# Two feed-forward networks over five token tiles in place of six, unrolled, with one buffer for the activated chunk

## The reference, cut to what matters

```python
def _attn_ref(q, k, v):                      # q, k, v: (4, 8, 1152, 64)
    q_pool = q.reshape(B, H, S // 2, 2, D).mean(axis=3)
    scores = scale * np.matmul(q_pool, k.transpose(0, 1, 3, 2))
    ...
    return np.matmul(attn, v)                # softmax over the keys

def _moe_ref(x, w_in, w_out):                # x: (2304, 512), w_in: (512, 2048)
    h = x @ w_in
    g = h * (1.0 / (1.0 + np.exp(-h)))
    return g @ w_out

def _moe2_ref(x, w1, w2, w3, w_out):         # w1, w2: (512, 1024), w3: (1024, 1024)
    a = x @ w1
    b = x @ w2
    h = a * b @ w3
    return h @ w_out                         # (2304, 512)
```

## Time and profile before

| | us |
|---|---|
| median of 3 runs | 1469.06 (1468.89 to 1470.64) |
| profiled execution: span from first to last instruction | 1465.5 |
| median less that span | 3.5 |
| TensorE busy | 1352.9 (92%) |
| VectorE busy | 799.6 (55%) |
| ScalarE busy | 697.3 (48%) |
| GpSimd busy | 434.8 (30%) |

### The profile page before, as it was taken

The page is one execution under the profiler, slowest core; times in us unless marked ns, Lnnn a source line. Parts: engine busy times, 40 slices in busy tenths (PEclk is TensorE's granted clock), DMA queues, the critical chain, the costliest instruction groups (busy, mean ns, idle before and its releaser), DMA issues.

```text
span 1465.5 us, 24978 instructions
## 1 busy us (share of the span) xinstructions
PE 1352.9 (92%) x8224; PEld 1296.8 (88%) x8224; DVE 799.6 (55%) x1340; ACT 697.3 (48%) x1266; POOL 434.8 (30%) x322
## 2 busy tenths in 40 slices
PE   6888888888888888889999999999999999999998
PEld 5887877787778787778899999999999899999998
DVE  7888888888888889888531111111114522122221
ACT  4776666666666666667742222222224422121211
POOL 4766656666655766655200000000000000000000
PEclk9999999999999999999999999999999999999999
DMA  6233323333323233320220000000104200000000
GB/s 155 73 81 81 95 64 80 81 79 81 91 68 81 68 92 81 79 72 24 61 65 8 1 1 1 1 0 0 43 0 153 92 1 22 23 22 1 21 21 22
DMA packets 33694, 76.34 MB, mean 52 GB/s; under 512 B 8944, under 2 KB 12144, under 8 KB 33648
## 3 DMA queue, kind: packets, MB, share of 16 engines
q1 hardware_dynamic: 33648, 75.73, 19.1%
HBM read 70.84 MB, written 4.79 MB: 52 GB/s over the span
## 4 chain that ended last, share of the span: by engine, by line
PE 77%; DVE 13%; issue 7%; DVEq 1%; DMA 1%; ACT 0%; SPq 0%; ACTq 0%
PE psum L907 21%; PE psum L908 20%; PE psum L909 20%; PE psum L923 5%; PE psum L924 4%; DVE mx L708 4%; PE psum L948 3%; PE psum L949 3%; DVE mneg L717 2%; DVE pL L726 2%; DVE mneg L719 2%; PE psum L932 1%; DVE kB L691 1%; DVE xT L732 1%; DVE qHs L702 1%
## 5 line engine op out<-in xcount | busy, mean ns | idle before, releaser
L708 DVE TENSOR_REDUCE mx<-psum 128x1 f32<-128x384 f32 (+1 forms) x480 | 253.1, 548 | 74.3 <-PE psum L924 73.7
L516 ACT ACTIVATE pF<-psum 128x576 f32<-128x576 f32 x288 | 187.7, 652 | 158.9 <-PE psum L949 156.8
L923 PE MATMUL psum<-kA,qHm 128*128 128x384 f32 (+1 forms) x480 | 172.4, 359 | 60.5 <-DVE mx L708 50.4
L836 DVE TENSOR_TENSOR gL<-gF,gH 128x384 fp32r<-128x384 f32 x96 | 53.6, 558 | 306.0 <-ACT gH L593 306.0
L424 POOL TENSOR_TENSOR pL<-pF,pH 128x576 fp32r<-128x576 f32 x93 | 143.0, 1538 | 216.8 <-ACT pH L522 216.7
L522 ACT CAST pH<-pF 128x576 fp32r<-128x576 f32 x288 | 194.5, 675 | 4.6
L726 DVE TENSOR_TENSOR pL<-pF,pH 128x576 fp32r<-128x576 f32 x195 | 187.6, 962 | 15.0 <-ACT pH L522 14.5
L907 PE MATMUL psum<-pH,vH 128*128 128x288 f32 x576 | 178.7, 310 | 1.5 <-DVE xT L732 0.7
L590 ACT ACTIVATE gF<-psum 128x384 f32<-128x384 f32 x96 | 47.3, 492 | 261.9 <-PE psum L909 261.9
L909 PE MATMUL psum<-pH,vL 128*128 128x288 f32 x576 | 171.0, 297 | 0.0
L908 PE MATMUL psum<-pL,vH 128*128 128x288 f32 x576 | 170.8, 297 | 0.0
(11 more groups left out here) (88 smaller groups left out, 3030.0 us busy)
## 6 DMA issues: line engine op xcount, KB each, us to landing
qraw<-in_qT SPq DMA_DIRECT2D x64, 288.0 KB, 4.2
kraw<-in_kT SPq DMA_DIRECT2D x64, 288.0 KB, 5.1
vraw<-in_v SPq DMA_DIRECT2D x32, 288.0 KB, 2.7
rsums<-recips SPq DMA_DIRECT2D x32, 144.0 KB, 2.9
outT<-oS SPq DMA_DIRECT2D x6, 768.0 KB, 3.4
wstage<-in_w_in SPq DMA_DIRECT2D x16, 256.0 KB, 3.4
fstage<-in_w3T SPq DMA_DIRECT2D x8, 512.0 KB, 4.7
w12stage<-in_w SPq DMA_DIRECT2D x8, 512.0 KB, 4.7
```

Of the source, the lines that this page charges most:

```text
L516: act.activation(two(pF[r][:]), stbank[(NC * j + c) % 2], ACT.Exp, scale=SCALE).then_inc(exp_done, 1)
L708: dve.tensor_reduce(mx[0:m, qt, b:b + 1], max_bank(h, jj, t)[0:m, 0:KW], AX.X, ALU.max)\
L923: pe.matmul(out, qHm[jj][:, cols], kA[jj][:, kblock(b)], start=True, stop=False)
```

## The change

The 2304 tokens are cut into five tiles: four of 464 columns and a last one of 448. All tile loops of both networks are written out, on all engines. `gF` has one buffer in place of two, so the silu of a chunk waits for the `gL` of the chunk before it. The order of the two `xH`, `xL` buffers is changed (the first network now begins with buffer 1), and `sums`, `rsums` and `ident` move into the memory of the attention stage; two waits are added for what now lies over them. The attention stage's instructions are the same.

```diff
-    TILE = 384
-    TILES = TOK // TILE
+    TILES = -(-TOK // 512)
+    TILE = -(-TOK // TILES // 16) * 16
...
-        ident = sb("ident", [P])
         wstage = sb("wstage", [WSLICE])
-        sums = sb("sums", [Q])
-        rsums = sb("rsums", [Q])
...
+            sums = sb("sums", [Q], F32, st)
+            rsums = sb("rsums", [Q], F32, st)
...
-        for j in range(2):
+        for j in (1, 0):
             xH[j] = sb(f"xH{j}", [KC, TILE], F32R, ffn)
             xL[j] = sb(f"xL{j}", [KC, TILE], F32R, ffn)
+            if j == 1:
+                with ExitStack() as st:
+                    fstage = [sb(f"fstage{r}", [FOLDW], F32, st) for r in range(2)]
...
-            gF = [sb(f"gF{r}", [TILE], F32, st) for r in range(2)]
+            gF = sb("gF", [TILE], F32, st)
...
+        def span(t):
+
+            return slice(t * TILE, min(TOK, (t + 1) * TILE))
+
+        def width(t):
+
+            return slice(0, min(TILE, TOK - t * TILE))
...
-            with sp.Fori(0, TILES // 2) as u:
-                for e in range(2):
-                    sp.wait_ge(out_taken, (2 * u + e + 1) * MC)
-                    sp.dma_start(out_v[:, :, bass.ds((2 * u + e) * TILE, TILE)], oS[e][:]
-                                 ).then_inc(out_stored[e], 16)
+            for t in range(TILES):
+                sp.wait_ge(out_taken, (t + 1) * MC)
+                sp.dma_start(out_v[:, :, span(t)], oS[t % 2][:, :, width(t)]).then_inc(out_stored[t % 2], 16)
...
+            act.wait_ge(qLm_ready, HEADS)
             act.wait_ge(normalized, HPB)
-            x_hi(0, 0, xH_ready, (h_ready, 0))
+            x_hi(0, 1, xH_ready, (h_ready, 0))
...
-            def silu(n, r):
+            def silu(n, r, w):
                 act.wait_ge(h_ready, n + 1)
-                need(act, gL_ready, n - 1)
-                act.activation(gF[r][:], hbank[r], ACT.Silu).then_inc(silu_done, 1)
+                need(act, gL_ready, n)
+                act.activation(gF[:, w], hbank[r][:, w], ACT.Silu).then_inc(silu_done, 1)
...
                         dve.wait_ge(woH_ready, c + 1)
+                        if c == C1 // 4:
+                            dve.wait_ge(normalized, PAIRS)
...
-            tile1(0, 0)
-            tile1(1, 1)
-            with pe.Fori(1, TILES // 2) as u:
-                tile1(2 * u, 0)
-                tile1(2 * u + 1, 1)
+            for t in range(TILES):
+                tile1(t, (t + 1) % 2)
             second1(TILES - 1, C1 - 1)
```

More of the change, by code:

```diff
@@ L117, in block_kernel @@
             identR = sb("identR", [P], F32R, st)
+            ident = sb("ident", [P], F32, st)
         ffn = ExitStack()
-        with ExitStack() as st:
-            fstage = [sb(f"fstage{r}", [FOLDW], F32, st) for r in range(2)]
         xH, xL = [None, None], [None, None]
-        for j in range(2):
+        for j in (1, 0):
             xH[j] = sb(f"xH{j}", [KC, TILE], F32R, ffn)
             xL[j] = sb(f"xL{j}", [KC, TILE], F32R, ffn)
+            if j == 1:
+                with ExitStack() as st:
+                    fstage = [sb(f"fstage{r}", [FOLDW], F32, st) for r in range(2)]
         with ExitStack() as st:
@@ L153, in block_kernel @@
         firstbank = [psum[:, r, :] for r in range(4)]
-        hbank = [psum[:, r, 0:TILE] for r in range(2)]
-        accbank = [psum[:, 2 + m, 0:TILE] for m in range(MC)]
-        abbank = [[psum[:, 0, 0:TILE], psum[:, 6, 0:TILE]], [psum[:, 1, 0:TILE], psum[:, 7, 0:TILE]]]
+        hbank = [psum[:, r, :] for r in range(2)]
+        accbank = [psum[:, 2 + m, :] for m in range(MC)]
+        abbank = [[psum[:, 0, :], psum[:, 6, :]], [psum[:, 1, :], psum[:, 7, :]]]
         FOLD_ORDER = [0, 6, 1, 7, 2, 3, 4, 5]
@@ L576, in x_hi @@
                 for k in range(KC):
-                    act.copy(xH[e][:, k, :], xT[:, k, bass.ds(t * TILE, TILE)]).then_inc(ready, 1)
+                    act.copy(xH[e][:, k, width(t)], xT[:, k, span(t)]).then_inc(ready, 1)
             act.wait_ge(kA_lo, KB * HEADS)
@@ L597, in take_y @@
                 for m in range(0, MC, 2):
-                    act.copy(xT[:, m, bass.ds(t * TILE, TILE)], accbank[m]).then_inc(y_taken, 1)
+                    act.copy(xT[:, m, span(t)], accbank[m][:, width(t)]).then_inc(y_taken, 1)
             act.wait_ge(*lo_done(HEADS - 1, NC - 1))
@@ L617, in tile1 @@
                         act.copy(woH[:, c, :], wostage[c % 2][:]).then_inc(woH_ready, 1)
-                    silu(C1 * t + c, c % 2)
+                    silu(C1 * t + c, c % 2, width(t))
                     if c == 0 and not first:
@@ L627, in tile1 @@
                         x_hi(t + 1, 1 - e, xH_ready, (h_ready, C1 * t))
[L629 to L635, removed]
+            for t in range(TILES):
+                tile1(t, (t + 1) % 2, t == 0, t == TILES - 1)
             take_y(TILES - 1)
@@ L658, in take_out @@
                 for m in range(0, MC, 2):
-                    act.copy(oS[e][:, m, :], accbank[m]).then_inc(out_taken, 1)
+                    act.copy(oS[e][:, m, width(t)], accbank[m][:, width(t)]).then_inc(out_taken, 1)
             def tile2(t, e, last):
@@ L665, in tile2 @@
                     need(act, pr_done, n - 1)
-                    act.copy(aS[r][:], abbank[r][0]).then_inc(a_copied, 1)
+                    w = width(t)
+                    act.copy(aS[r][:, w], abbank[r][0][:, w]).then_inc(a_copied, 1)
                     act.wait_ge(pr_done, n + 1)
                     need(act, pr_used, n - 1)
-                    act.copy(prH[r][:], pr[r][:]).then_inc(prH_ready, 1)
+                    act.copy(prH[r][:, w], pr[r][:, w]).then_inc(prH_ready, 1)
                     if c == C2 // 2 and not last:
@@ L673, in tile2 @@
                         take_out(t - 1, 1 - e)
[L675 to L682, removed]
+            for t in range(TILES):
+                tile2(t, t % 2, t == TILES - 1)
+            take_out(TILES - 1, (TILES - 1) % 2)
         @block.vector
@@ L803, in x_lo @@
                     dve.wait_ge(hi_ready, KC * t + k + 1)
-                    dve.tensor_tensor(xL[e][:, k, :], xT[:, k, bass.ds(t * TILE, TILE)], xH[e][:, k, :].bitcast(F32),
+                    dve.tensor_tensor(xL[e][:, k, width(t)], xT[:, k, span(t)], xH[e][:, k, width(t)].bitcast(F32),
                                       ALU.subtract).then_inc(ready, 1)
-            x_lo(0, 0, xH_ready, xL_ready)
+            x_lo(0, 1, xH_ready, xL_ready)
             take_o(HEADS - 1, PAIRS - 1, 1)
@@ L815, in take_y @@
                 for m in range(1, MC, 2):
-                    dve.tensor_copy(xT[:, m, bass.ds(t * TILE, TILE)], accbank[m]).then_inc(y_taken, 1)
+                    dve.tensor_copy(xT[:, m, span(t)], accbank[m][:, width(t)]).then_inc(y_taken, 1)
             def fold_lo(c):
@@ L1012, in first1, with second @@
                     cols = slice(k * FF + c * P, k * FF + (c + 1) * P)
-                    last = three(hbank[c % 2], winH[:, cols], winL[:, cols], xH[e][:, k, :], xL[e][:, k, :],
-                                 start=(k == 0), stop=(k == KC - 1))
+                    last = three(hbank[c % 2][:, width(t)], winH[:, cols], winL[:, cols], xH[e][:, k, width(t)],
+                                 xL[e][:, k, width(t)], start=(k == 0), stop=(k == KC - 1))
                 last.then_inc(h_ready, 1)
-            def second(hi, lo, wH, wL, c, chunks):
+            def second(hi, lo, w, wH, wL, c, chunks):
                 for m in range(MC):
                     cols = slice(m * P, (m + 1) * P)
-                    last = three(accbank[m], wH[:, c, cols], wL[:, c, cols], hi[:], lo[:],
+                    last = three(accbank[m][:, w], wH[:, c, cols], wL[:, c, cols], hi[:, w], lo[:, w],
                                  start=(c == 0), stop=(c == chunks - 1))
@@ L1030, in second1 @@
                     need(pe, y_taken, MC * t)
-                second(gH[c % 2], gL[c % 2], woH, woL, c, C1).then_inc(g_used, 1)
+                second(gH[c % 2], gL[c % 2], width(t), woH, woL, c, C1).then_inc(g_used, 1)
             def tile1(t, e):
@@ L1077, in first2 @@
                         cols = slice(g * F2 + c * P, g * F2 + (c + 1) * P)
-                        last = three(abbank[c % 2][g], w12H[:, k, cols], w12L[:, k, cols], xH[e][:, k, :],
-                                     xL[e][:, k, :], start=(k == 0), stop=(k == KC - 1))
+                        last = three(abbank[c % 2][g][:, width(t)], w12H[:, k, cols], w12L[:, k, cols],
+                                     xH[e][:, k, width(t)], xL[e][:, k, width(t)], start=(k == 0), stop=(k == KC - 1))
                 last.then_inc(ab_ready, 1)
@@ L1087, in second2 @@
                         pe.wait_ge(foldL_ready, C2)
-                second(prH[c % 2], prL[c % 2], foldH, foldL, c, C2).then_inc(pr_used, 1)
+                second(prH[c % 2], prL[c % 2], width(t), foldH, foldL, c, C2).then_inc(pr_used, 1)
             def tile2(t, e):
@@ L1096, in tile2 @@
                         second2(t - 1, C2 - 1)
[L1098 to L1102, removed]
```

(2 more changed lines are left out.)

16 lines of the change are left out of this document (10 added, 6 removed).

## The result

The changed kernel takes 1471.88 us (median of 20 runs, 1469.57 to 1473.43), the kernel before 1469.09 in the same series: ratio 1.0019, 95% interval 1.0012 to 1.0026. It is a little slower, where 1460.0 was forecast.

What follows compares the result with a forecast made beforehand. Both networks were taken as bound by back-to-back TensorE matmuls; -8.96 - 0.54 + 0.47 = -9.03 us takes the span from 1465.5 to 1456.5, and 3.5 us between span and median gives 1460.0 us, range 1457.0 to 1464.0.

Steps and rivals of the forecast that it cites:

- Step 1: Both networks: five tiles for six means 672 fewer matmuls, each with a fixed price of about 13.3 ns: -8.96 us.
- The rival of blocks of 32: TensorE takes columns in blocks of 32, so 464 costs as 480: +17.9 us, 1477.9 us, slower; chance 5%.
- Price by columns: Matmul price goes by columns, N x 0.4514 ns, so five tiles cost what six do: 1469.0 us, same; chance 3%.
- The Trainium skill's N / 2.4 + 2.5 ns: Fixed part per matmul only 2.5 ns: the 672 fewer would save only 1.7 us, time 1467.3 us.
- Step 2: Start of first network: TensorE's first wait, 0.54 us for gL, vanishes with 464 columns: -0.54 us, between -0.54 and 0.
- Steps 3 to 5: Both networks: wider ACT and VectorE work, one gF buffer, and new waits for moved buffers all stay covered: zero each.
- step 5: New waits for moved buffers cost zero; chunk 2's woL deadline, met by some 0.2 us, gets about 1.7 us of slack.
- Step 6: Unrolling, one more tile body of straight code per network: zero, between -0.2 and +0.5 us.
- Step 7: Kernel end: last chunk's chain -0.07, two VectorE copies +0.14, larger output transfer +0.4: together +0.47 us.
- Step 8: Attention keeps its instructions, only some addresses change: zero, but one half-clock stretch more or less is worth at most 1.7 us.
- The clock: Rival: the clock falls because the TensorE array is fuller, 93.5% of the time streaming for 92.3%; slower, chance 1%.

## Why the prediction was wrong

**Step 1 failed, and by it alone the sign.** It put the price of 464 columns between those of 384 and 512, "where the fixed part is 13.3 and 13.4", and the bounds of the range came from the same rows. The two widths that fix that line, 384 and 512, were both widths that pay nothing extra at their places, with blocks 1536 and 2048 bytes apart. At 464 columns 3.3 to 3.4 ns come on top at 2048-byte places and about 3.9 at 1856 bytes, at 448 2.2 there in the bare matmuls and 3.5 in the kernel. The fewer matmuls brought their 8.96 us, and the dearer ones took 12.8. How much of the 12.8 is the width's and how much the places', the runs don't separate in the changed kernel; the bare matmuls have both. The 288 row had the hint in it: 132.7 ns where the line has 133.3, and its distances, 127 to 136 ns, weren't even. I took it as a bound of a fixed price; it was a sign that the price isn't fixed. An interpolation in the width also left out that the change moves the moving blocks to other places against their weights, which nothing in the prediction prices; at 384 columns that alone cost 6.7 us. With widths that do lie on the line, the same number of matmuls brought 8.9 us.

**The rival of blocks of 32** had the right sign and the right point of decision, 210.0 ns at 464 columns; the measured 210.6 is just beyond it. Its mechanism is wrong: 448 and 480 are multiples of 32 and were dear in the kernels.

**Price by columns**: refuted by the five tiles of 512 and 384, which gained 8.9 us. The Trainium skill's N / 2.4 + 2.5 ns (TensorE: Matmul & The Clock Gate, "Wait - 56ns, not 53.3ns?") doesn't hold here: the lowest mean that the bare matmuls paid above N / 2.4 is 11.7 ns, at 288 columns. Had it held, the kernel of 512 and 384 would have gained 1.7 us.

**Step 2**, right: no wait for gL in the changed kernel. The first silu began 2.8 us after the network's first matmul, as before, and gL ended 4.65 us after it, where 4.8 was reckoned and TensorE came at about 5.0. **Steps 3 to 5**, right: no wait for gL or woL in the changed kernel, and the kernel with six tiles and these parts stands at 0.9995. Its one new wait, at chunk 2, shows how thin the slack of step 5 was at 384 columns. The wait for the last normalisation was met: POOL ended it at 727.4, and VectorE's woL of chunk 4 started at 734.55. **Step 6**, right: 0.9998. **Step 7**, right in its parts: VectorE's last two copies went from 1.02 to 1.15 us and the last transfer from 3.4 to 3.8. From the last matmul's start to the end of the span it is 5.77 us for 5.39.

```profile
1464.11 1.15 DVE L874 COPY oS<-psum 128x448 f32<-128x448 f32 x2 [2.80 <-PE psum L904]
...
outT<-oS SPq DMA_DIRECT2D x1, 896.0 KB, 3.8
```

**Step 8**, right in kind: attention ended between 716.6 and 719.0 us in the eight full profiles, for kernels that all leave its instructions alone; the changed kernel's 717.4 is within that. **The clock** stayed at 1.00 in both networks and the fold, so this rival falls.

Two figures of the prediction don't follow from its terms. The second network to the end should have read 301.8 us and not 300.9 (305.2 - 3.84 + 0.47), and 13.4 ns by 672 matmuls bounds step 1 at -9.0, not -9.1; neither bears on the forecast. And 3.5 us were taken to lie between span and time. For the profiled run of the changed kernel, span 1469.5 and time 1471.3, it is 1.8. If the same lies around the profiled run before, that one took 1467.3 us and was among the faster ones, and the other 1.7 us would be differences from run to run.

## What to carry to other kernels

A pitch read at one width holds for that width at those addresses. Before widths or buffer sizes change, measure the new width with the new spacing in a kernel of bare matmuls: 96 matmuls at 464 columns and 1856 bytes showed the 210.5 ns that decided this case. For fp32r products with a weight load each, 384 and 512 columns with moving blocks and weights at the same place modulo 256 bytes paid nothing extra, in the bare matmuls and in the kernel; 256, 320 and 352 did so in the bare matmuls alone. Here unequal tiles (512 and 384) beat nearly equal ones (464 and 448) by 0.7%, with the same number of matmuls.

## What the runs showed of the hardware

A matmul of fp32r with its own weight load cost N / 2.4 GHz + 13.3 ns from start to start at 256, 320, 352, 384 and 512 columns with good places (120.0, 146.7, 160.0, 173.3 and 226.7 ns), and up to 6.7 ns more at other places. All widths tried from 416 to 504 paid more with blocks 2048 bytes apart, 1.7 to 9.0 ns. Leaving 80 unused columns between blocks cost 6.7 us in all, 2.9 ns for each matmul that reads them. 504 columns cost as much as 512 (226.7 ns), and 288 cost 1.7 ns less than the line.
